# The first chunk of a gated linear attention with two MLPs: loads on two queues, masks by ScalarE and GpSimd, weights converted in place

## What is computed

```python
def _attn_ref(q, k, v, alpha):
    state = np.zeros((B, H, D, D)); y = np.zeros_like(q)
    for t in range(S):
        state = alpha[:, :, t, :, None] * state + np.einsum('bhd,bhe->bhde', k[:, :, t], v[:, :, t])
        y[:, :, t] = np.einsum('bhd,bhde->bhe', q[:, :, t], state)
    return y

x = attn.transpose(0, 2, 1, 3).reshape(B * S, H * D)
x = (np.maximum(x @ w_in, 0) ** 2) @ w_out            # first MLP
h = x @ w2_in; x = (h * (1 / (1 + np.exp(-h)))) @ w2_out   # second MLP
```

## Time and profile before

| | us |
|---|---|
| median of three runs | 951.12 (948.94 to 951.31) |
| the profiled execution | 952.14 |
| its span | 950.5 |
| PE busy | 916.7, 96% of the span |
| DVE busy | 449.2, 47% |
| ACT busy | 403.4, 42% |
| POOL busy | 81.2, 9% |
| granted TensorE clock, mean | 0.989 of 2.4 GHz |

### The profile page before, as it was taken

How to read it: one execution, slowest core, us unless ns; L and a number is a source line. 1 busy time by engine, 2 the same in 40 slices (tenths; PEclk the granted TensorE clock), 3 DMA queues, 4 the chain that set the end, 5 groups by cost and what they waited for, 6 DMA issues and landing times.

```text
span 950.5 us, 12762 instructions
## 1 busy us (share of the span) xinstructions
PE 916.7 (96%) x4822; PEld 764.8 (80%) x4822; DVE 449.2 (47%) x684; ACT 403.4 (42%) x744; POOL 81.2 (9%) x119
## 2 busy tenths in 40 slices
PE   5668999999999999999999999999999999999997
PEld 5657888888888888888888888888888888888897
DVE  5578888667777766667334421221311312212310
ACT  3335455445444544454466653322333323333520
POOL 6633320000000000000013300000000000000000
PEclk9798999999999999999999999999999999999999
DMA  9834443422332342231033310110110100200100
GB/s 185 199 102 114 108 119 78 108 61 61 94 76 68 77 114 64 61 95 21 14 103 97 101 67 1 34 33 1 34 34 1 54 13 1 67 1 1 33 9 28
DMA packets 97235, 60.09 MB, mean 63 GB/s; under 512 B 55824, under 2 KB 87184, under 8 KB 97168
## 3 DMA queue, kind: packets, MB, share of 16 engines
q1 hardware_dynamic: 92928, 46.53, 20.0%
q0 software_dynamic: 4096, 12.59, 4.6%
q10 hardware_dynamic: 144, 0.10, 0.0%
HBM read 45.02 MB, written 9.44 MB: 57 GB/s over the span
## 4 chain that ended last, share of the span: by engine, by line
PE 94%; DVE 2%; issue 1%; DMA 1%; ACT 0%; SPq 0%; POOL 0%; DVEq 0%; POOLq 0%
PE h_ps L531 41%; PE z_ps L544 39%; PE job_ps L562 3%; PE job_ps L483 3%; PE job_ps L516 3%; PE job_ps L512 2%; PE job_ps L500 1%; PE job_ps L489 1%; PE z_ps L562 1%; DMA w_raw<-in_moe_w_out 1%; DVE rcp L841 1%; PE job_ps L455 0%; PE h_ps L568 0%; SPq L289 0%; DMA nat_a<-in_alpha 0%
## 5 line engine op out<-in xcount | busy, mean ns | idle before, releaser
L908 DVE TENSOR_TENSOR g_lo<-g,g_hi 128x512 fp32r<-128x512 f32 x177 | 124.2, 702 | 317.9 <-ACT g_hi L713 242.9
L531 PE MATMUL h_ps<-x_hi,win_hi 128*128 128x512 f32 x576 | 225.1, 391 | 7.9 <-ACT g L710 4.9
L531 PE MATMUL h_ps<-x_lo,win_hi 128*128 128x512 f32 x576 | 224.7, 390 | 0.0
L531 PE MATMUL h_ps<-x_hi,win_lo 128*128 128x512 f32 x576 | 224.6, 390 | 0.0
L708 ACT ACTIVATE g<-h_ps 128x512 f32<-128x512 f32 x96 | 57.5, 599 | 232.0 <-PE h_ps L531 232.0
L710 ACT ACTIVATE g<-h_ps 128x512 f32<-128x512 f32 x96 | 57.4, 598 | 199.3 <-PE h_ps L531 175.6
L531 PEld LDWEIGHTS h_ps<-x_hi,win_hi 128*128 128x128 f32 x576 | 108.5, 188 | 30.9 <-issue 8.4
L531 PEld LDWEIGHTS h_ps<-x_lo,win_hi 128*128 128x128 f32 x576 | 108.6, 189 | 22.6
L531 PEld LDWEIGHTS h_ps<-x_hi,win_lo 128*128 128x128 f32 x576 | 108.5, 188 | 22.6
L544 PE MATMUL z_ps<-g_hi,wout_hi 128*128 128x512 f32 x288 | 118.5, 411 | 0.0
L713 ACT ACTIVATE g_hi<-g 128x512 fp32r<-128x512 f32 x177 | 111.8, 632 | 5.6
(11 more groups left out here) (126 smaller groups left out, 938.4 us busy)
## 6 DMA issues: line engine op xcount, KB each, us to landing
w_raw<-in_moe_w_in POOLq DMA_DIRECT2D x32, 192.0 KB, 3.0
w_raw<-in_moe_w_out POOLq DMA_DIRECT2D x32, 192.0 KB, 3.1
v_sb<-in_v SPq DMA_DIRECT2D x48, 96.0 KB, 2.7
z_scratch<-z_sb SPq DMA_DIRECT2D x18, 256.0 KB, 2.5
x_raw<-z_scratch SPq DMA_DIRECT2D x6, 768.0 KB, 4.5
out_x<-z_sb SPq DMA_DIRECT2D x80, 48.0 KB, 1.7
nat_a<-in_alpha SPq DMA_DIRECT2D x40, 88.0 KB, 2.2
nat_k<-in_k SPq DMA_DIRECT2D x40, 88.0 KB, 2.2
```

The lines of the kernel that those rows point to most:

```text
L531: last = nc.tensor.matmul(h_ps[f % 2][:], w[:, f, tile(kk)], x[par][:, kk, :], start=(kk == 0 and n == 0), stop=(kk == KD - 1 and n == 2))
L908: nc.vector.tensor_tensor(low, g[f % 2][:], high.bitcast(F32), ALU.subtract).then_inc(g_lo_made, 1)
```

## The change

- **Loads.** The first twelve loads (alpha, k and q of pairs 0 and 1, two heads each) are issued by SP for one head and by ACT for the other, at the head of their queues. "KQ" in the list becomes "K" and "Q", in new places.
- **Masks.** For pairs 0 to 2 ACT copies the scores out of PSUM (`s_copy`) and POOL applies the mask with an affine_select in place (`mask`). DVE masks pair 3 and all later ones as before.
- **Bounds.** ACT's two squares are issued apart: the decay's as soon as it is scanned, the reciprocal's later. DVE's scaling of q waits for the first alone.
- **Decay end.** POOL copies it for pairs 0 to 3.
- **Banks.** Alpha is turned into `z_ps0` and `z_ps1` in turn, k into `h_ps0`, q into `job_ps1`; the I products go to `z_ps2`, `h_ps1`, `z_ps0`, `z_ps1`.
- **State.** `first_state` makes the state of pairs 0 to 3 from PSUM in one instruction a head, without `inc`.
- **Weights.** The first MLP's weights are loaded in four groups of DMAs (blocks 0 to 1, 2 to 5, 6 to 10, 11 to 15; three DMAs for `w_in` and one for `w_out` each) into `win_raw` and `wout_raw`, which occupy the place of `win_lo` and `wout_lo`: the subtraction writes over its input. 12 chunks are rounded ahead of the main loop, the other 20 in steps 0 to 9, two a step. The group loads, masks, pads and subtractions stand in a written-out order on POOL.
- **First products.** `keep_warm` is gone. The first two of three tiles of F = 0 and 1 (12 matmuls) stand ahead of the main loop, and x is split tile by tile.
- **Later pairs.** Pair 4 has its stages at steps 0, 2, 3, 4, 4 instead of -1, 1, 2, 3, 3, and pairs 5 to 7 follow three steps apart; from pair 8 on nothing is moved.

The diff, cut to its core:

```diff
-AHEAD = [("A", 0), ("A", 1), ("KQ", 0), ("S", 0), ("A", 2), ("KQ", 1), ("I", 0), ("Y", 0), ("S", 1), ("A", 3),
-         ("KQ", 2), ("I", 1), ("Y", 1), ("S", 2), ("KQ", 3), ("I", 2), ("Y", 2), ("S", 3), ("I", 3), ("Y", 3), ("A", 4)]
-FIRST_PE = {0: 6, 1: 8, 2: 8, 3: 4}
-WARM_AFTER = 24
+AHEAD = [("A", 0), ("A", 1), ("K", 0), ("Q", 0), ("S", 0), ("K", 1), ("A", 2), ("I", 0), ("Q", 1), ("Y", 0),
+         ("S", 1), ("K", 2), ("A", 3), ("I", 1), ("Q", 2), ("Y", 1), ("S", 2), ("K", 3), ("I", 2), ("Q", 3), ("Y", 2),
+         ("S", 3), ("I", 3), ("Y", 3)]
+WGROUPS = [(0, 2), (2, 6), (6, 11), (11, 16)]
+EARLY_CHUNKS = 12
-        return {"A": -1, "KQ": 1, "S": 2, "I": 3, "Y": 3}[kind] + 3 * (n - PAIRS)
+        return {"A": 0, "KQ": 2, "S": 3, "I": 4, "Y": 4}[kind] + 3 * (n - PAIRS)
...
+        wout_hi = sb("wout_hi", [P, NF, DM], F32R)
+        with ExitStack() as arrival:
+            win_raw = sb("win_raw", [P, NF, DM], F32, arrival)
+            wout_raw = sb("wout_raw", [P, NF, DM], F32, arrival)
         win_lo = sb("win_lo", [P, NF, DM], F32R)
-        wout_hi = sb("wout_hi", [P, NF, DM], F32R)
         wout_lo = sb("wout_lo", [P, NF, DM], F32R)
...
+        def a_bank(n):
+            return z_ps[n % 2]
         def i_bank(n):
-            return early_ps[n] if n < PAIRS else job_ps[1]
+            return [z_ps[2], h_ps[1], z_ps[0], z_ps[1]][n] if n < PAIRS else job_ps[1]
...
+        def first_raw(n):
+            return (wout_raw if n % 2 else win_raw)[:, n // 2, :]
...
-            for kind in "akq":
-                load_nat(kind, 0)
-            for kind in "akq":
-                load_nat(kind, 1)
+            for n in (0, 1):
+                for kind in "akq":
+                    load_head(sp, kind, 0, n, 0, nat[kind][n][:, :, :, 0:HD], nat_in[kind][n])
...
+            def ends(n):
+                pool.wait_ge(scanned, BATCH * (n + 1))
+                nc.gpsimd.tensor_copy(decay_end[:, n, :], qp[n % 2][:, P - 1::P]).then_inc(end_made, 1)
+            def mask(n):
+                for h in (0, 1):
+                    pool.wait_ge(s_copied, 2 * n + h + 1)
+                    nc.gpsimd.affine_select(out=score[h][:], in_=score[h][:], compare_op=ALU.is_ge, fill=0.0,
+                                            base=0, pattern=[[0, BATCH], [1, P]], channel_multiplier=-1).then_inc(masked, 1)
+            def load_first(i):
+                f0, f1 = WGROUPS[i]
+                for kk in range(KD):
+                    pool.dma_start(win_raw[:, f0:f1, tile(kk)],
+                                   w1_in[tile(kk), f0 * P:f1 * P].rearrange("p (f n) -> p f n", n=P)).then_inc(w1_arrived[0][i], 16)
+                pool.dma_start(wout_raw[:, f0:f1, :], w1_out[f0 * P:f1 * P, :].rearrange("(f p) d -> p f d", p=P)
+                               ).then_inc(w1_arrived[1][i], 16)
+            def low_first(n):
+                hi, lo = chunk(n)[:2]
+                pool.wait_ge(w_hi_made, n + 1)
+                nc.gpsimd.tensor_tensor(lo, first_raw(n), hi.bitcast(F32), ALU.subtract).then_inc(w_lo_made, 1)
+            ends(0)
+            pool.wait_ge(nat_in["q"][1], 32)
+            load_first(0)
             nc.gpsimd.memset(state[:], 0.0).then_inc(pads, 1)
+            ends(1)
+            mask(0)
             for n in "akq":
                 for i in range(2):
                     nc.gpsimd.memset(nat_sb[n][i][:, :, LOADED:LOADED + 16], 1.0 if n == "a" else 0.0).then_inc(pads, 1)
-            for n in range(RING):
-                load_chunk(n, chunk(n)[2], n)
-            for n in range(NCHUNK):
-                hi, lo = chunk(n)[:2]
-                pool.wait_ge(w_hi_made, n + 1)
-                nc.gpsimd.tensor_tensor(lo, w_raw[n % RING][:], hi.bitcast(F32), ALU.subtract).then_inc(w_lo_made, 1)
-                load_chunk(n, chunk(n + RING)[2], n + RING)
-            for n in range(NCHUNK + RING, 2 * NCHUNK):
+            load_first(1)
+            ends(2)
+            mask(1)
+            low_first(0)
+            low_first(1)
+            ends(3)
+            mask(2)
+            for n in range(2, 8):
+                low_first(n)
+            load_first(2)
+            load_first(3)
+            for n in range(8, NCHUNK):
+                low_first(n)
+            for n in range(NCHUNK, 2 * NCHUNK):
...
-                turn("a", n, early_ps[n]).then_inc(a_made, 1)
-            def kq_stage(n):
+                wait(pe, scanned, BATCH * (n - 1))
+                turn("a", n, a_bank(n)).then_inc(a_made, 1)
+            def k_stage(n):
                 loaded("k", n)
-                wait(pe, kt_copied, n)
-                turn("k", n, job_ps[0]).then_inc(k_made, 1)
+                wait(pe, k_scaled, n)
+                turn("k", n, h_ps[0]).then_inc(k_made, 1)
+            def q_stage(n):
                 loaded("q", n)
-                wait(pe, masked, 2 * n - 1)
+                wait(pe, s_copied, 2 * n - 1)
                 turn("q", n, job_ps[1]).then_inc(q_made, 1)
...
-            def keep_warm(n):
-                for _ in range(n):
-                    nc.tensor.matmul(h_ps[0][:, 0:P], ident[:], causal[:], start=True, stop=True)
             pe.wait_ge(consts, CONSTS)
             for kind, n in AHEAD:
-                if kind == "S":
-                    keep_warm(FIRST_PE[n])
                 stage(kind, n)
-            keep_warm(WARM_AFTER)
+            pe.wait_ge(k_scaled, PAIRS)
+            pe.wait_ge(state_made, 2 * 2)
+            for f in (0, 1):
+                pe.wait_ge(w_lo_made, 2 * f + 1)
+                first_product(0, 0, f, win_hi, win_lo, range(KD - 1))
             for F in range(2 * STEPS):
                 u, f = divmod(F, NF)
-                if F == 1:
-                    wait(pe, inc_made, 2 * PAIRS)
...
-                    first_product(u, u % 2, f, win_hi, win_lo)
+                    first_product(u, u % 2, f, win_hi, win_lo, range(KD - 1, KD) if F < 2 else range(KD))
                 else:
                     first_product(u, u % 2, f, win2_hi, win2_lo)
...
-                        wait(pe, inc_made, 2 * PAIRS)
+                        wait(pe, state_made, 2 * PAIRS)
...
+            def bound_decay(n):
+                wait(act, scanned, BATCH * (n + 1))
+                nc.scalar.activation(square[:], qp[n % 2][:], ACT.Square, accum_out=bound[:, n, 0:1]).then_inc(bound_made, 1)
+            def bound_reciprocal(n):
                 wait(act, rcp_made, 2 * (n + 1))
-                nc.scalar.activation(square[:], qp[n % 2][:], ACT.Square, accum_out=bound[:, n, 0:1]).then_inc(bound_made, 1)
                 wait(act, bound_made, 2 * n + 1)
                 nc.scalar.activation(square[:], rcp, ACT.Square, accum_out=bound[:, n, 1:2]).then_inc(bound_made, 1)
                 wait(act, bound_made, 2 * n + 2)
+            def s_copy(n):
+                wait(act, y_made, n)
+                wait(act, s_made, n + 1)
+                for h in (0, 1):
+                    nc.scalar.activation(score[h][:].rearrange("s b t -> s (b t)"), job_ps[1 + h][:], ACT.Copy).then_inc(s_copied, 1)
...
+                group = [f0 <= n // 2 < f1 for f0, f1 in WGROUPS].index(True)
+                wait(act, w1_arrived[n % 2][group], 16 if n % 2 else 16 * KD)
+                nc.scalar.activation(hi, first_raw(n), ACT.Copy).then_inc(w_hi_made, 1)
...
+            def split_first_x(kk):
+                for p in (kk, kk + 1):
+                    wait(act, y_moved[p % 2], moved(0, p + 2))
+                split_x_tile(0, kk)
...
+            for n in (0, 1):
+                for kind in "akq":
+                    load_head(act, kind, 0, n, 1, nat[kind][n][:, :, :, 0:HD], nat_in[kind][n])
-            for n in range(PAIRS):
-                bounds(n)
-                for c in range(5 * n, 5 * n + 3):
-                    split_chunk(c)
-                kt_copy(n)
-                for c in range(5 * n + 3, 5 * n + 5):
-                    split_chunk(c)
-                y_copy(n)
-            split_x(0, ys=1)
-            bounds(PAIRS)
+            bound_decay(0)
+            bound_reciprocal(0)
+            for n in range(1, PAIRS):
+                s_copy(n - 1)
+                bound_decay(n)
+                kt_copy(n - 1)
+                split_chunk(2 * n - 2)
+                bound_reciprocal(n)
+                split_chunk(2 * n - 1)
+                y_copy(n - 1)
+            kt_copy(PAIRS - 1)
+            split_first_x(0)
+            split_chunk(6)
+            split_chunk(7)
+            split_first_x(1)
+            y_copy(PAIRS - 1)
+            for c in range(8, EARLY_CHUNKS):
+                split_chunk(c)
+            split_first_x(2)
             for F in range(2 * STEPS):
                 u, f = divmod(F, NF)
                 step(u, f, g_pair(F)[0], u >= UNITS)
                 if u < UNITS:
                     square_g(f)
-                if u == 0 and EARLY_CHUNKS + f < NCHUNK:
-                    split_chunk(EARLY_CHUNKS + f)
+                if u == 0:
```

(38 more changed lines are left out.)

63 lines of the change are left out of this document (32 added, 31 removed).

## The result

The changed kernel takes 943.53 us (median of eight runs, 943.19 to 945.11), the kernel before 950.39 beside it: ratio 0.9937 (95% interval 0.9919 to 0.9955). It is faster by 0.6%, and not by the 2.1% that was forecast; 943.53 lies outside the range 925 to 940. In the profiled executions it is 952.14 against 945.11: 7.0 us, of 20.1 predicted. Executions of one kernel differ: the profiled one of the changed kernel is the slowest of its eight, 1.6 us above their median, and that of the kernel before lies 1.8 above its own.

A forecast was written before the change was run, and what follows sets the result against it. TensorE bounds from about 80 us, so the question was how much earlier that state comes: 17.8 at pair 4's scores plus 4.1 of matmuls done, less 1.8, gives 20.1 off 952.14, 932.0, or 931 as median; range 925 to 940.

The forecast's parts named there:

- The cycle: Pairs before the main loop: a closed chain of PE and ACT in turn takes 7.2 us a pair, the first 8.5.
- the 0.5 taken for the second queue: Start: SP and ACT issuing six head loads each brings PE's first turn 0.5 us earlier, at 3.95.
- the three ends weighed: POOL's mask, no row at this size: 0.6, 1.16 or 1.35 us a head; free up to some 1.9.
- The crowding at F = 14: Pair 7's state update, pair 8's k and q crowd on DVE; they end about 1.0 us after PE reaches the scores.
- "Covered": SP's strictly ordered queue: pair 4's alpha ahead of pair 3's q and pair 0's repack was claimed to cost nothing.
- "PE never pauses for more than 1.5 us": New pair cycle: PE's pauses stay within 1.5 us, the argument against the clock staying at 1.2 GHz.
- one of the signs of being wrong: Listed signs: mask over 1.9 us, granted clock 0.50 between 20 and 36, ACT's weight wait over 4, PE's F = 14 wait over 2.
- rival (1): Without fillers the clock stays at 1.2 GHz: cycle 10.0, 7 us lost there and 1 in the tail, 939; chance 0.15.
- the tail's 4.3 us for the landing of rows: After pair 3's y copy: 4.3 us until the repacked rows land and x's last split starts, at 44.4.
- Rival (3): Last rows land late because 3.9 MB of weights start at the same instant: three to six us more, 936; chance 0.10.
- to the mark: From x's last tile through pair 4's alpha chain, 5.97, to the start of its scores: 60.0 against 77.81.
- the half clock behind pair 4's scores: After PE's long pause, scores, transposes and some seven matmuls run at half clock: 0.8 us lost.

The follow-up runs named there:

- rows first: Changed kernel with SP's 24 loads of alpha, k and q for pairs 4 and 5 issued behind the repack of pair 3: 942.2 us, ratio 0.9903.
- the groups early: Changed kernel with weight group 2 issued behind the mask of pair 1 and group 3 behind that of pair 2: 948.58 us, ratio 0.9987.
- the masks on VectorE: Changed kernel with the masks of pairs 0 to 2 back on VectorE, without ScalarE copy or GpSimd mask: 948.65 us, ratio 0.9978.
- all together: Changed kernel with later loads behind SP's rows, weight group 2 earlier, group 3 held, pair 4's transpose and scan before x's last tile: 934.13 us, ratio 0.9835.
- the run with fillers: Changed kernel with constant matmuls put back, 24 behind the early products and 28 in step 3: 942.07 us, ratio 0.9913.
- weights held: Changed kernel with GpSimd issuing weight groups 2 and 3 only when the last pair's rows have landed in x: 940.8 us, ratio 0.9903.
- alpha ahead: Changed kernel with pair 4's alpha stage on VectorE and its squares on ScalarE ahead of x's last tile: 939.0 us, ratio 0.9881.

## Why the prediction was wrong

**What held.** The cycle was forecast at 7.2 and came at 7.18, in part by luck (the clock, two paragraphs below), and its first at 8.1 instead of 8.5. Pair 0's scores came at 11.86 against 11.45: the first turn started at 4.36, so of the 0.5 taken for the second queue 0.1 came. These two misses of 0.4 cancel. The mask costs 0.61 a head (two in 1.22), the lower of the three ends weighed, and is free. The crowding at F = 14 costs 1.24 (the lead rises there by 2.86 with 18 matmuls, 4.1, more done before) against 1.0. The pause before pair 4's scores, forecast 6.7, was 7.6. Weight group 2 had landed when ACT came to its first chunk (58.37).

**Failed: "Covered", of SP's queue.** I had followed SP for what its loads wait for and to when the loads themselves are wanted, and not for what stands behind them: 24 loads, the repack of each pair and v. Four grouped loads took 3.30 and 3.44 us to issue (23.04, 26.44), where 1.7 to 2.0 is usual, and v took up to 9.4 us to land. Price: 0.7 of wait for v in the cycle into pair 3, and 2.7 because the late rows of pair 2 held ACT in front of the last y copy. In the run with rows first the i product does not wait, and the last y copy ends at 39.84, against 40.1 forecast.

**Failed in part: "PE never pauses for more than 1.5 us".** It paused 2.20 and 2.04, and the granted clock was 0.50 at 21 to 24 and at 32 to 34 us, one of the signs of being wrong that the prediction names. The rest of the 1.7 into pair 3 is this: that cycle took 8.98 where the run with the rows first, with the clock at 1.00, took 6.76, and 1.5 of the difference is half clock. The cycle before took 7.18 against 6.70. So rival (1) came for 2.0 us of its 7, and the chain itself is 0.45 shorter than I had added up, which half clock hid. The clock went either way without an edit: in the run where POOL waits for the scan, the same code up to 41 us, PE paused only 0.79 before pair 1's scores and the clock stayed at 1.00 to 32 us.

**Failed: the tail's 4.3 us for the landing of rows.** It was a row of a quiet stretch of before, used for a place where I had myself put 3.9 MB at the same instant. Rival (3) named the mechanism but priced it with three to six for the rows alone and 0.10. It was 4.7 there, and in other runs it worked at two more places: on v (the groups early) and on the rows of pair 2 (the masks on VectorE, all together). The price came from a load of 192 KB among twelve (4.2), not from the queue of bytes in front: at the 310 GB/s of 48 to 54 us those 3.9 MB alone are 12.6 us of full DMA engines, an upper end that I could have given from the earlier trace rows too (17 at 230).

**Mis-sized: to the mark.** 2.9 us: the scan of pair 4 took 3.58 instead of 1.37 (2.2), and the last three first products ran at half clock after a pause of 6.3, 1.6 instead of 0.7 (0.9), less 0.2 in the rest. That POOL's subtractions would stand beside this scan could be read from the order of the change; I had taken the duration of a scan that had no such neighbour.

**Mis-sized: the half clock behind pair 4's scores.** The lead falls by 1.64 between the scores of pairs 4 and 5 (5.79 to 4.15), where 0.8 was forecast. Half clock cost 3.2 there by the run with fillers; that half of it does not show in the lead is since the kernel before also took 18.36 us between these two, and not 16.80: its granted clock was 0.64 from 78 to 81 us and 0.96 from 81 to 96. The prediction had looked at its scores alone.

**What stays open.** The parts of the account are differences of instants in one execution of each kernel, and the executions of one kernel differ by 2 us and more. How far the runs lie below the changed kernel (us) depends on what is compared:

| run | profiled executions | medians | ratios to the kernel before |
|---|---|---|---|
| weights held | 5.1 | 2.7 | 3.2 |
| rows first | 3.7 | 1.3 | 3.2 |
| alpha ahead | 6.5 | 4.5 | 5.3 |
| all together | 13.2 | 9.4 | 9.7 |

The signs agree and the sizes do not: the late transfers (the first two runs) are worth 8.7 by the first column, 4.1 by the second and 6.5 by the third, where the account gives them 9.1. What differs between executions of one kernel no run shows. Nor is it settled why the rows of a pair in the burst are split 7.0 us after their issue in one kernel and 10.0 in another; the bytes in flight ahead of them differ, and no run varies these alone.
